# Attention with nine query tiles per pair of heads: one unrolled order, the division moved behind the product with V, operands split on GpSimd

## The reference

```python
# attention: B, H, S, D = 2, 8, 1152, 64; q pooled by 2 along the sequence
q_pool = q.reshape(B, H, S // factor, factor, D).mean(axis=3)
scores = scale * np.matmul(q_pool, k.transpose(0, 1, 3, 2))
scores = scores - np.max(scores, axis=-1, keepdims=True)
attn = np.exp(scores)
attn = attn / (np.sum(attn, axis=-1, keepdims=True) + 1e-09)
return np.matmul(attn, v).astype(np.float32)
...
# its output, as 1152 tokens of 512, goes through two expert stages
for e in range(E):                        # E = 4, all tokens
    h = np.maximum(x @ w1[e], 0.0)
    out += p[:, e:e + 1] * (h @ w2[e])
...
expert_idx = np.argmax(logits, axis=1)    # 8 experts, each token to one of them
```

## Time and profile before

| | us |
|---|---|
| median of 3 runs | 1005.42 |
| lowest, highest | 1002.42, 1006.47 |
| span of the profiled execution | 1002.8 |
| attention, first scores to the end of the last half of O | 15.4 to 381.7 |
| first expert stage, about | 384 to 788 |
| second expert stage, from its first matmul | 828 to the end |

### The profile page before, as it was taken

How to read it: one execution, slowest core, us unless ns; L and a number is a source line. 1 busy time by engine, 2 the same in 40 slices (tenths; PEclk the granted TensorE clock), 3 DMA queues, 4 the chain that set the end, 5 groups by cost and what they waited for, 6 DMA issues and landing times.

```text
span 1002.8 us, 14755 instructions
## 1 busy us (share of the span) xinstructions
PE 879.9 (88%) x4740; PEld 753.5 (75%) x4741; DVE 511.9 (51%) x901; ACT 435.0 (43%) x794; POOL 285.1 (28%) x166
## 2 busy tenths in 40 slices
PE   2888888888888879999999999999999709999996
PEld 2666666666666768898989898989898607878885
DVE  4788888888878854141414141314131322299225
ACT  4677777777777643030303031303131502278224
POOL 3766667766667521000000000000000040133112
PEclk9999999999999979999999999999999858999998
DMA  8333222234227221010201120012000062197510
GB/s 263 83 83 84 71 59 59 59 81 95 59 59 185 75 85 52 33 49 37 84 1 32 53 84 0 22 62 84 1 1 1 0 235 70 42 308 255 209 42 23
DMA packets 30095, 79.66 MB, mean 79 GB/s; under 512 B 4008, under 2 KB 4008, under 8 KB 30065
## 3 DMA queue, kind: packets, MB, share of 16 engines
q1 hardware_dynamic: 27104, 70.58, 23.9%
q0 software_dynamic: 2960, 8.68, 2.7%
HBM read 69.52 MB, written 10.78 MB: 80 GB/s over the span
## 4 chain that ended last, share of the span: by engine, by line
PE 76%; ACT 7%; issue 6%; DVE 6%; DMA 3%; POOL 1%; SPq 1%; ACTq 0%; POOLq 0%; DVEq 0%
PE L L337 20%; PE L L400 20%; PE ring L322 7%; PE L L505 7%; PE L L479 6%; PE ring L309 4%; PE scores L290 4%; PE scores L291 3%; ACT a L550 2%; DVE aTl L700 2%; ACT aTh L514 2%; PE ring L307 1%; DMA xr<-sorted_rows 1%; ACT o_vl L514 1%; POOL sorted_rows L1069 1%
## 5 line engine op out<-in xcount | busy, mean ns | idle before, releaser
L1021 POOL TENSOR_TENSOR a<-a,rinv 128x1152 f32<-128x1152 f32 (+1 forms) x80 | 168.5, 2106 | 106.2 <-DVE rinv L754 104.1
L700 DVE TENSOR_TENSOR aTl<-ring,aTh 128x384 fp32r<-128x384 f32 (+1 forms) x240 | 118.5, 512 | 62.0 <-ACT aTh L514 60.6
L309 PE MATMUL ring<-ident,a 128*128 128x128 f32 (+1 forms) x672 | 110.4, 277 | 37.1 <-ACT o_vl L514 18.2
L514 ACT ACTIVATE aTh<-ring 128x384 fp32r<-128x384 f32 (+1 forms) x240 | 106.5, 458 | 70.9 <-PE ring L309 66.3
L619 ACT ACTIVATE hh<-L 128x384 fp32r<-128x384 f32 x96 | 46.6, 491 | 204.2 <-PE L L337 204.2
L337 PE MATMUL L<-xTh,w1h 128*128 128x384 f32 x384 | 131.2, 342 | 4.4 <-DVE hl L832 2.3
L337 PE MATMUL L<-xTl,w1h 128*128 128x384 f32 x384 | 130.8, 341 | 0.0
L337 PE MATMUL L<-xTh,w1l 128*128 128x384 f32 x384 | 130.6, 340 | 0.0
L1069 POOL DMA_INDIRECT sorted_rows<-acc,posi x9 | 10.7, 1186 | 415.0 <-DVE posi L924 412.6
L309 PEld LDWEIGHTS ring<-ident,a 128*128 128x128 f32 (+1 forms) x672 | 75.4, 145 | 64.9 <-DVE aTl L700 32.8
L832 DVE SCALAR_TENSOR_TENSOR hl<-L,hh 128x384 fp32r<-128x384 f32 x96 | 52.8, 557 | 125.4 <-ACT hh L619 125.4
(11 more groups left out here) (155 smaller groups left out, 1580.6 us busy)
## 6 DMA issues: line engine op xcount, KB each, us to landing
raw<-in_v SPq DMA_DIRECT2D x48, 512.0 KB, 5.9
raw<-in_w SPq DMA_DIRECT2D x32, 512.0 KB, 5.2
rawK<-in_kT SPq DMA_DIRECT2D x32, 288.0 KB, 5.1
rawQ<-in_qT SPq DMA_DIRECT2D x32, 288.0 KB, 5.8
sorted_rows<-filler SPq DMA_DIRECT2D x19, 257.0 KB, 9.4
rawV<-in_vr SPq DMA_DIRECT2D x16, 288.0 KB, 5.9
xr<-sorted_rows POOLq DMA_DIRECT2D x15, 257.0 KB, 3.0
out<-o,destc POOLq DMA_INDIRECT x13, 2.8
```

What stands on the lines that cost most here:

```text
L309: last = pe.transpose(o, src, ident[0:m, 0:m])
L514: return act.activation(o, i, ACT.Copy, **kw)
L700: return dve.tensor_tensor(o, i0, i1, op)
L1021: pool.tensor_tensor(a[t][0:m, :], a[t][0:m, :], rinv[0:m, t:t + 1].to_broadcast([m, SEQ]), ALU.mult).then_inc(S["norm_ready"], 1)
```

## The change

A pair has nine tiles: four of the first head, one mixed tile (`XT`) that holds the last 64 queries of both heads, four of the second. The mixed tile's scores are four matmuls per chunk, over Q operands padded with zeros in 64 columns (`AW`). All 72 steps are written out on every engine, without loops.

The tile isn't multiplied by the reciprocal of its sum any more: the exp is transposed as it is, and y is divided after the product with V. VectorE forms the reciprocals of a pair at once (`rinv_pair`), GpSimd spreads them over columns (`spread_pair`), TensorE transposes those in two turns N of the ring, steps 4 and 6 of the next pair (`spread_rinv`), and VectorE multiplies (`normalize`).

Round 0 of a tile goes to the first chunk's bank of its own scores buffer, so the ring carries rounds 1 and 2, halves of O and the turns N. Scores are made two tiles ahead instead of four, chunks 2 and 1 between rounds 0 and 1, chunk 0 behind round 2; the exp is one tile ahead and there are three tile buffers. The half of O stands at the end of the step. On VectorE round 2 of tile g-1 follows round 0 of tile g, then comes the max of tile g+2, then round 1 of tile g. GpSimd rounds and splits K, Q, V (but for head 0) and y, and adds the pieces of O. K and Q are loaded apart from V.

```diff
-TPH = len(QT)
-TPP = 2 * TPH
+FULL = QS // P
+XW = QS - FULL * P
+TPP = 2 * FULL + 1
+XT = FULL
...
+HALF = QS // 2
+V_STEP = {(0, 0): 3, (0, 1): 5, (1, 0): 8, (1, 1): TPP + 1}
+N_STEP = (4, 6)
...
+        a = [sb(f"a{i}", [P, SEQ], F32, att) for i in range(3)]
+        aTh = sb("aTh", [P, KT_N, AW], F32R, att)
+        aTl = sb("aTl", [P, KT_N, AW], F32R, att)
...
         turns = []
-        for k in range(TPP):
-            turns += [("T", k, 0)]
-            turns += [("V", k, 1)] * (k % TPH == V_TILES[1]) + [("V", k, 0)] * (k % TPH == V_TILES[0])
-            turns += [("T", k, 1), ("T", k, 2)]
-        assert len(turns) % 2 == 0
+        for g in range(TPP * PAIRS):
+            j, k = g // TPP, g % TPP
+            turns += [("T", g, 1), ("T", g, 2)]
+            for (s, u), step in V_STEP.items():
+                if step % TPP == k and j >= step // TPP:
+                    turns += [("V", v_index(j - step // TPP, s, u), 0)]
+            if k in N_STEP and j:
+                turns += [("N", j - 1, N_STEP.index(k))]
+        turns += [("V", v_index(PAIRS - 1, 1, 1), 0), ("N", PAIRS - 1, 0), ("N", PAIRS - 1, 1)]
+        place = {turn: i for i, turn in enumerate(turns)}
...
+            return ring[place[turn] % 2]
+        def given_back(turn):
+            kind, i, r = turn
             if kind == "T":
-                return S["a_lo"], RPT * (TPP * j + k) + i + 1
-            return S["o_taken"], 2 * (2 * j + k // TPH - (i == 1)) + i + 1
...
+                return S[f"a_lo{r}"], i + 1
+            if kind == "V":
+                return S["o_taken"], i + 1
+            return S[("y_main", "y_ready")[r]], i + 1
...
+        def bank_free(eng, turn):
+            if place[turn] >= 2:
+                eng.wait_ge(*given_back(turns[place[turn] - 2]))
...
+            o = scores[g % 2][:, 0, 0:SW] if r == 0 else bank(("T", g, r))[:, 0:KPR * P]
...
+            for n in range(2, NH):
+                s = n % 2
+                sp.wait_ge(S["k_lo"], n - 1)
+                sp.wait_ge(S["q_sum"], n - 1)
+                load_kq(n, s)
+                sp.wait_ge(S["v_lo"], n - 1)
+                load_v(n, s)
...
+                for c in chunks:
+                    if c == 0:
+                        at_least(pe, S["a_lo0"], g - 1)
...
+            def times_v(j, s, u):
+                pe.wait_ge(S["a_lo2"], TPP * j + ((2, 4), (7, 8))[s][u] + 1)
+                pe.wait_ge(S["a_lo1"], TPP * j + ((2, 4), (7, 8))[s][u] + 1)
+                pe.wait_ge(S["v_lo"], 2 * j + s + 1)
+                turn = ("V", v_index(j, s, u), 0)
+                bank_free(pe, turn)
+                c0 = s * XW + u * HALF
...
+            def spread_rinv(j, part):
+                pe.wait_ge(S["spread_ready"], 2 * (j + 1))
+                turn = ("N", j, part)
+                bank_free(pe, turn)
+                for i, t in enumerate((range(FULL), (XT,))[part]):
+                    last = pe.transpose(bank(turn)[:, i * P:(i + 1) * P], spread[:, t * P:(t + 1) * P], ident[:])
+                last.then_inc(S["nb_ready"], 1)
...
+            for g in range(TPP * PAIRS):
+                j, k = g // TPP, g % TPP
+                transpose_round(g, 0)
+                if g + 2 < TPP * PAIRS:
+                    score_part(g + 2, (2, 1))
+                transpose_round(g, 1)
+                transpose_round(g, 2)
+                if g + 2 < TPP * PAIRS:
+                    score_part(g + 2, (0,))
+                for (s, u), step in V_STEP.items():
+                    if step % TPP == k and j >= step // TPP:
+                        times_v(j - step // TPP, s, u)
+                if k in N_STEP and j:
+                    spread_rinv(j - 1, N_STEP.index(k))
+            pe.wait_ge(S["x_lo"], PAIRS - 1)
+            pe.wait_ge(S["exp_ready"], TPP * PAIRS)
+            pe.wait_ge(S["a_lo0"], TPP * PAIRS)
+            for f in range(2):
+                up_tile(0, 0, f)
+            times_v(PAIRS - 1, 1, 1)
+            spread_rinv(PAIRS - 1, 0)
+            spread_rinv(PAIRS - 1, 1)
+            for f in range(2, L1_BANKS):
+                up_tile(0, 0, f)
...
+            exp_tile(0)
+            for g in range(TPP * PAIRS):
+                j, k = g // TPP, g % TPP
+                split_hi(g, 0)
+                if g + 1 < TPP * PAIRS:
+                    exp_tile(g + 1)
+                for (s, u), step in V_STEP.items():
+                    if (step + 1) % TPP == k and j >= (step + 1) // TPP:
+                        take_o(j - (step + 1) // TPP, s, u)
+                split_hi(g, 1)
+                split_hi(g, 2)
...
+            max_tile(1)
+            for g in range(TPP * PAIRS):
+                j, k = g // TPP, g % TPP
+                split_lo(g, 0)
+                if g:
+                    split_lo(g - 1, 2)
+                if k - 1 in N_STEP and j:
+                    normalize(j - 1, N_STEP.index(k - 1))
+                if g + 2 < TPP * PAIRS:
+                    max_tile(g + 2)
+                if k == 1 and j:
+                    rinv_pair(j - 1)
+                split_lo(g, 1)
+                if j == PAIRS - 1 and k in EARLY_PARTS:
+                    weights_lo(0, 1, EARLY_PARTS[k])
+            split_lo(TPP * PAIRS - 1, 2)
+            rinv_pair(PAIRS - 1)
+            dve.wait_ge(S["o_taken"], 4 * PAIRS)
...
+            def prep_k(n, s):
+                p = n // 2
+                at_least(pool, S["s_ready"], (TPP * (p - 1) + (XT + 1, TPP)[s]) if p else 0)
+                pool.wait_ge(S[f"kq_in{s}"], 64 * (p + 1))
+                pool.tensor_copy(KT[s][:], rawK[s][:]).then_inc(S["k_hi"], 1)
...
+            def prep_q(n, s):
+                cols = slice(0, QS) if s == 0 else slice(XW, AW)
+                pool.wait_ge(S["q_lo"], n)
+                pool.wait_ge(S["k_lo"], n + 1)
+                pool.tensor_tensor(qs[:], rawQ[s][:, 0, :], rawQ[s][:, 1, :], ALU.add).then_inc(S["q_sum"], 1)
+                pool.wait_ge(S["q_sum"], n + 1)
+                pool.tensor_scalar(qs[:], qs[:], SCALE, None, ALU.mult).then_inc(S["q_scaled"], 1)
+                pool.wait_ge(S["q_scaled"], n)
+                pool.tensor_copy(QTh[s][:, cols], qs[:]).then_inc(S["q_hi"], 1)
+                pool.wait_ge(S["q_hi"], n + 1)
+                pool.tensor_tensor(QTl[s][:, cols], qs[:], QTh[s][:, cols].bitcast(F32), ALU.subtract) \
+                    .then_inc(S["q_lo"], 1)
...
+            def add_o(j):
+                pool.wait_ge(S["o_taken"], 4 * (j + 1))
+                at_least(pool, S["y_ready"], j)
+                pool.tensor_tensor(ysum[:], o_vh[:], o_vl[:], ALU.add).then_inc(S["ysum_ready"], 1)
...
+            for j in range(PAIRS):
+                if j:
+                    add_o(j - 1)
+                    spread_pair(j - 1)
+                prep_v(2 * j + 1, 1)
+                if j + 1 < PAIRS:
+                    prep_k(2 * j + 2, 0)
+                    prep_q(2 * j + 2, 0)
+                if j:
+                    split_x(j - 1)
+                if j + 1 < PAIRS:
+                    prep_v(2 * j + 2, 0)
+                    prep_k(2 * j + 3, 1)
+                    prep_q(2 * j + 3, 1)
+            spread_pair(PAIRS - 1)
```

More of the change, by code:

```diff
@@ L278, in _ @@
         def _(pe):
-            def score_tile(n, s, t, g):
-                if t == 0:
-                    pe.wait_ge(S["k_lo"], n + 1)
-                    pe.wait_ge(S["q_lo"], n + 1)
-                at_least(pe, S["exp_ready"], g - 1)
-                q0, m = QT[t]
-                b = (5 * s + t) % 2
-                for c in range(SC):
-                    keys = slice(c * SW, (c + 1) * SW)
-                    o = scores[b][0:m, c, 0:SW]
-                    pe.matmul(o, QTh[s][:, q0:q0 + m], KT[s][:, keys], start=True, stop=False)
-                    last = pe.matmul(o, QTl[s][:, q0:q0 + m], KT[s][:, keys], start=False, stop=True)
-                last.then_inc(S["s_ready"], 1)
@@ L294, in transpose_round, with score_part @@
-            def transpose_round(t, k, r, j, g, first):
-                m = QT[t][1]
+            def score_part(g, chunks):
+                j, k = g // TPP, g % TPP
+                if g == XT:
+                    pe.wait_ge(S["pads_ready"], 4)
+                if k == 0 or k == XT:
+                    pe.wait_ge(S["k_lo"], 2 * j + (k == XT) + 1)
+                    pe.wait_ge(S["q_lo"], 2 * j + (k == XT) + 1)
+                at_least(pe, S["exp_ready"], g - 1)
+                heads = ((0, X_COLS[0]), (1, X_COLS[1])) if k == XT else \
+                    ((tile_head(k)[0], q_cols(*tile_head(k))),)
+                for c in chunks:
+                    if c == 0:
+                        at_least(pe, S["a_lo0"], g - 1)
+                    keys = slice(c * SW, (c + 1) * SW)
+                    n = 0
+                    for s, cols in heads:
+                        for Q in (QTh, QTl):
+                            last = pe.matmul(scores[g % 2][:, c, 0:SW], Q[s][:, cols], KT[s][:, keys],
```

(19 more changed lines are left out.)

386 lines of the change are left out of this document (140 added, 246 removed).

## The result

| | before | after |
|---|---|---|
| median, us | 1005.88 | 1159.59 |
| lowest, highest | 1002.42, 1006.47 | 1157.38, 1160.33 |
| span of the profiled execution | 1002.8 | 1157.3 |
| first transposes | 28.1 | 19.7 |
| one pair of heads in attention | 44.3 | 64.9 |

The changed kernel is slower by a ratio of 1.154 [1.152, 1.156], 154 us. The prediction was 1138 with a range from 1085 to 1188. Attention ends 152 us later, so nearly the whole difference lies there.

What follows compares the result with a forecast made beforehand. It took a loop of bank waits through several engines, none full, as the bound: span 1002.8 us plus 93 (attention's waits, start, end) plus 39 (clock) is 1135, median 2.6 above, so 1138; range 1085 to 1188.

Steps and rivals of the forecast that it cites:

- The chain: Attention: TensorE's next instruction waits for a bank that other engines empty late; a pair takes 56.9 us, against 44.3 before.
- a plain step: Attention step without a half of O or reciprocals' transposes: 3.72 us, no faster than the 3.45 of before.
- S: Start of the chunk-0 scores of tile g+2, the point from which the forecast counts each attention step.
- the steps with a half: Four attention steps per pair that hold a half of O, which waits for VectorE's max: 8.40 us each.
- The clock's term: Attention: gaps ahead of halves of O and reciprocal steps lower TensorE's clock, adding 39 us (bounds 0 and about 96).
- Start and end: First transposes at about 19.8 us, tile 2's chunk-0 scores at 22.6; serial end to the fifth up tile some 26 us.
- the end of the cover: Attention: GpSimd's 29 us of work per pair would no longer be hidden if a pair took under 35 us.
- TensorE under 60% busy: Sign to look for in attention's busy table, together with pairs of 57 us or more.
- The full clock: Rival: bank waits slow attention as forecast but TensorE's clock stays at 1.00; 1098 us, chance 0.26.
- The mostly low clock: Rival: bank waits as forecast and TensorE's clock low for most of attention; 1194 us, chance 0.07.
- Faster: Rival: banks come back before TensorE needs them, its own work bounds a pair at 34 to 37 us; 931 us, chance 0.08.
- GpSimd as the bound: Rival: GpSimd copies at two to three times the assumed cost, over 57 us per pair; 1162 us at 65, chance 0.04.

Runs made afterwards that it cites:

- mended order: Changed kernel with all its parts, instructions reordered on TensorE, ScalarE (copies of O ahead of exp) and VectorE (three subtractions ahead of the max): 961.49 us, ratio 0.957.

## Why the prediction was right, and where its sizes were off

**The chain held.** The prediction's term for a pair at full clock, 56.9 us, came out as 57.0 in the kernel with filled gaps, and its steps too: in after 3.75 for a plain step (forecast 3.72; S at 271.29 and 275.04), 2.60 from S to the half (2.57), 3.28 from the half to the next S (3.32); with the gaps filled 8.3 to 8.4 between maxima for three of the steps with a half (8.40), 9.07 for the fourth, which has the small reciprocals (8.70), and 6.1 and 5.6 for the reciprocals' (6.1 and 5.4). The causes named held too: the half starts 1.4 us earlier when VectorE's subtraction goes first, and the copies of O ahead of the exp bring 22 us, some 6 of them by the clock. What made this possible was taking the order of the new program and the durations of the old trace, and not the busy times: by those alone (the removed tile, the removed multiplications) one would have forecast a gain.

**The clock's term was too small.** Forecast 39 us (bounds 0 and 96), measured 62. I took 1.5 us for two thirds of the halves and 8 us for the rest. The 1.5 was right (3.95 less 2.5 is 1.45), the two thirds were not: in the pair that I read all four halves ran mostly at the low clock. That is 31 x 1.45 = 45 us. All 30 halves behind a gap bear it out: 3.98 us on average, and 2.49 with the gaps filled. The rest is 17 us, not 8: the pair of 64.86 us is 7.9 over 57.0, of which the halves are 5.8, so about 2 a pair lies elsewhere: 1.4 in the reciprocals' steps (6.62 and 6.45 between maxima, 6.1 and 5.6 with the gaps filled), the rest around them and the halves. This term alone carries the miss: 1138 + 23 = 1161 against 1159.6. My argument that a half at the end of attention brought the clock back within itself was one case, with gaps of about 1 us before it; here each gap was 2.0 us or more. The upper bound was added up too high as well: 31 x 1.9 and 72 x 0.45 make 91 us and not 96.

**Start and end.** First transposes 19.66 (19.8), S of tile 2 at 21.48 (22.6); from the last S at 510.29 to the fifth up tile at 538.98 it is 28.7 us (26), 2 us of it by the half at 522.12, which took 4.46 us. These errors are one to three microseconds each and in part cancel.

**GpSimd.** Forecast 29 us a pair, hidden. Measured 26.4 by the groups of after by shape:

```profile
L993 POOL TENSOR_TENSOR KT<-rawK,KT 64x1152 fp32r<-64x1152 f32 x15 | 39.3, 2622 | 1.2
...
L1002 POOL TENSOR_SCALAR qs<-qs 128x576 f32<-128x576 f32 x15 | 24.8, 1651 | 1.3
...
L991 POOL CAST KT<-rawK 128x1152 fp32r<-128x1152 f32 x15 | 17.2, 1145 | 9.3 <-DMA rawQ<-in_qT 7.8 <-PE scores L326 1.6
...
L1004 POOL CAST QTh<-qs 128x576 fp32r<-128x576 f32 x15 | 10.0, 665 | 1.0
```

(Columns: busy us, mean ns of one, idle before.) A copy of 1152 columns took 1.15 us, where I had taken 1.8 from between 1.2 and 2.1, so it fell just below the lower bound. I had put the end of the cover at 35 us a pair with 29 us of work. The mended order bears out that there is such an end: at 38.8 us a pair 26.4 us of work don't show among TensorE's waits, and 37 us of work cost 44 us in all.

**TensorE under 60% busy** was a wrong sign to look for: it is 69% (41.5 of 60). A matmul at the low clock is busy for longer. With the gaps filled, the filler is 1.75 x 6 = 10.5 us of a pair of 57, which leaves 46.5 - 11 of 60, or 59%: the forecast was right for the full clock only.

**The rivals.** The full clock (1098, chance 0.26) would have been right had the gaps been filled: 1097.7. The mostly low clock (1194) was too far: rounds and scores that follow a half ran mostly at full speed (clock 0.97 from 295 to 300 us, 1.00 from 312.4 to 316, 0.98 from 332.6 to 337). Faster (931) was excluded by the order of instructions, as argued; with another order it comes within 31 us of that figure (961). GpSimd as the bound (1162) gives almost the measured time, and the time alone couldn't have told it from the truth; the added memsets did (3 us for 80). Its condition was mis-sized too: by the prediction's own terms the copies and scalings are about 11 us of the 29 a pair, so that at three times their value GpSimd's work is some 51 us and not over 57.

## What to carry to other kernels

Before instructions are moved between queues, write down for each step who empties the buffer that the next instruction in order needs, and what stands ahead of the emptying on its engine; above all, an instruction that empties a bank never belongs behind one that waits for the very engine that wants the bank. Here one VectorE line in the wrong place cost 131 us, and the same change with a mended order is 4% faster than the kernel before. A gap on TensorE is priced twice, once as waiting and once as slow matmuls after it, and filling the gap with useless matmuls is a quick way to measure the second part apart from the first.

## What the hardware showed unexpectedly

- The clock often fell not in the gap but in the half behind it: in the half at 503.01 the first four matmuls start 0.13 to 0.22 us apart (to 503.49) and the later ones 0.24. In 20 of the 30 halves behind a gap it fell so, at most 0.9 us after the start. In the other ten the low clock was there from the first matmul, and in most of these it ended before the half did. Timeline of after, the first two matmuls of such a half, 0.38 us apart:

```profile
292.01 0.58 PE L354 MATMUL ring<-aTh,VV 128*128 128x288 f32 x1 [2.01 <-DVE aTl L712]
292.39 0.45 PE L354 MATMUL ring<-aTl,VV 128*128 128x288 f32 x1
```

- In either case a dense group pays for the gap ahead of it. The gap alone doesn't settle it: in the kernel with the copies first one half behind a gap of 2.01 us took 2.44 us, and with the subtraction first five of 30 halves were slow behind 0.6 us.
- 528 useless matmuls (74.7 us busy) made the kernel 62 us faster.
- On GpSimd, scaling 576 columns by a constant took 1.65 us, a cast of as many 0.67, a sum or difference of two operands 1.41. The Trainium skill, "GPSIMD Engine Reference", section Engine selection, calls work with one input roughly line-rate and with two about twice as slow as VectorE. For the casts the trace agrees (ScalarE took 0.69 for the same cast in the kernel before), and for two inputs too (VectorE took 0.75 for the same sum there, GpSimd 1.42); the scaling by a constant, also with one input, is dearer than the sum of two, and there the measurement decides.
